# Splitting the gate, up and down pieces of early tiles between runs of small products in a delta-rule attention kernel with two expert layers

## Chip, cores and metric
The kernel runs on one core of one Trainium2 chip. The metric is the device time of one execution in microseconds. Engines: PE is TensorE, ACT ScalarE, DVE VectorE, POOL GpSimd, SP SyncE, which issues the DMAs. PEld is PE's weight load.

## What is computed
The reference has three stages, and the change touches the stretch in which the first and the second overlap.

```python
# attention: batch 4, heads 8, sequence 768, head width 48
y[t] = q[t] @ state
state = state + beta[t] * outer(k_n[t], v[t] - state^T k_n[t])
# first expert layer: x [3072, 384], 8 experts, inner width 1024
P = sinkhorn(exp(x @ w_gate - max))            # 8 rounds
out = sum_e P[:, e] * (relu(x @ w1[e]) @ w2[e])
# second layer: inner width 2048
h = out @ w_in;  result = (h * cos(h)) @ w_out
```

## The kernel before
**Attention.** The sequence is worked in 6 groups (g = 0 to 5) of 4 steps (c = 0 to 3, called step 0 to step 3 here); a step takes 64 positions of 8 heads and 2 batches. Groups 0 to 2 are one pair of batches, 3 to 5 the other, so the state starts anew in group 3. A step on PE (`step`, L645) is a list of runs of small products (32 or 64 products each), written out by hand: `L657` keys by state, then `L681` the correction (needs the residual R from DVE, L1530), `L482` query products of the next step, `L698` queries by state (needs W, which ACT copies at L976), `L704` the state update (ACT copies it at L1036 as S), `L709` the outputs (ACT copies them at L1045 as yT). In some steps merges of triangular blocks, `L492` and `L495`, 64 small products each, are called as well (`merge`, L499); their results are copied by ACT at L1003 (Y1) and L1007 (X). The last step of groups 2 and 5 has no L704, the first of groups 0 and 3 no L657 and no L698.

**Triangular inverses.** DVE works the inverse of the blocks of a later group column by column (`leaf`, L1465, lines L1479 and L1481), in every step but step 2, where it turns the result with two transposes (L1523, L1524) and then the next group's blocks (L1457). DVE's stream is in order: in step 3 it is R and the mask (L1538), `early_lo(g-1, 1)`, the norms and the leaf's start (L1423 to L1463), `early_lo(g-1, 2)`, and only then the columns of the leaf; R of the next step stands behind those.

**Early tiles.** From group 1, step 2 on, PE also works the first expert's first half for the tile of 512 tokens that the group before has finished, in pieces of large products (128x128 by 512): up pieces j = 0 to 3 (`early_up`, L551, 9 products), the gate (`early_gate`, L567, 9), and down pieces d = 0 to 2 (`early_down`, L585, 12). Where they stand is written out in three functions: `beside_residual` (L610, between L657 and L681), `beside_update` (L631, called at L684 after L482 and ahead of the merges) and `beside_outputs` (L638, after L709). After an up piece ACT makes hhi (L1062) from the bank, DVE makes hlo (L1547) from both, and only then is the one bank h_ps free for the next up piece. Up piece j of tile g-1: j = 0 in step 2, j = 1 and 2 in step 3, j = 3 in step 0 of the next group.

Of ACT's stream the lines L1165 to L1173 count: in steps 2 and 3 the copies hhi (j = 0, or j = 2) come ahead of the merge's copy X, of S and of yT.

**After it.** The early tiles end at 325 us, and from there to the end (the other expert passes and the second layer, L771 on) PE works through large products alone.

Of the kernel before, what the change touches and what calls it, by code (L numbers as in the profile page):

```python
# [77 lines left out]
def build(nc, kta, kqt, krow, vrow, brow, wcat, wgate, out):  # L78
# [371 lines left out]
    def _(pe):  # L450
# [100 lines left out]
        def early_up(t, j):  # L551
            if j == 0:
                pe.wait_ge(o["x_done"], t + 1)

                pe.wait_ge(s["wlo_done"], NT // 2)

            pe.wait_ge(o["h_done"], t * CH + j)
            if t == 0 and j == 0:

                pe.wait_ge(a["a_evac"], 4 * NG)  # L560
            for d in range(DC):
                pe.matmul(h_ps[:, :], w1(whi, 0, d, j), xt_hi[:, d, :], start=(d == 0), stop=False)
                pe.matmul(h_ps[:, :], w1(whi, 0, d, j), xt_lo[:, d, :], start=False, stop=False)
                mm = pe.matmul(h_ps[:, :], w1(wlo, 0, d, j), xt_hi[:, d, :], start=False, stop=(d == DC - 1))
            mm.then_inc(o["up_done"], 1)

        def early_gate(t):  # L567
# [4 lines left out]
            for d in range(DC):  # L572
# [3 lines left out]
            mm.then_inc(o["gate_done"], 1)  # L576
# [8 lines left out]
        def early_down(t, d):  # L585
            if d == 0:
                pe.wait_ge(o["h_done"], (t + 1) * CH)

                pe.wait_ge(s["wlo_done"], NT)
# [9 lines left out]
            for j in range(CH):  # L599
# [3 lines left out]
            mm.then_inc(o["down_done"], 1)  # L603
# [26 lines left out]

        def beside_update(g, c):  # L631

            if g >= 1 and c == 2:
                early_up(g - 1, 0)
            if g >= 1 and c == 3:
                early_up(g - 1, 2)

        def beside_outputs(g, c):  # L638

            if g >= 2 and c == 0:  # L640
                early_gate(g - 2)
            if g >= 2 and c == 1:
                early_down(g - 2, 1)

        def step(g, c):  # L645
# [38 lines left out]
            beside_update(g, c)  # L684
# [8 lines left out]
            if c == 3 and g + 1 < NG:  # L693
                merge(g + 1, 1)
            pe.wait_ge(a["w_evac"], i + 1)
# [4 lines left out]
            if not last:  # L700
# [5 lines left out]
                mm.then_inc(a["ku_done"], 1)  # L706
            pe.wait_ge(a["p_evac"], i + 1)
# [211 lines left out]
    def _(act):  # L919
# [215 lines left out]
        for g in range(NG):  # L1135
            near, far = g + 1 < NG, g + 2 < NG
            for c in range(STEPS):
# [25 lines left out]
                elif c == 0:  # L1163
                    merged(g, 3)
                if c == 2 and g >= 1:  # L1165
                    early_hi(g - 1, 0)
                if c == 3:
                    if g >= 1:
                        early_hi(g - 1, 2)
                    if near:  # L1170
                        merged(g + 1, 1)
                state(g, c)
# [725 lines left out]
```

## Time and profile before

| what | us |
|---|---|
| median of 3 runs | 2217.0 |
| lowest, highest | 2215.49, 2217.49 |
| the profiled execution | 2215.68 |
| its span | 2213.9 |
| PE busy in it | 2169.7 (98%) |
| DVE, ACT, POOL busy | 1019.6, 702.7, 507.2 |
| granted TensorE clock, mean | 0.985 |

The profiled execution took 1.3 us less than the median; 1.8 us of it lie around its span. Of the span the stretch from 118.5 us (the first early up piece) to 311.6 us (the last attention product) is the one that holds the instructions that the change moves. In a timeline row the columns are start, duration, engine, line, operation, output and inputs, shape, count, and in brackets the idle time before and what ended it; "issue" there means that the engine waited for nothing that the profile shows.

### The profile page before, as it was taken

The page shows a single profiled execution, that of the slowest core. Times are in us where ns is not written, and L with a number is a line of the kernel's source. Part 1 is how long each engine was busy: PE and PEld are TensorE (multiplying, and loading weights), DVE is VectorE, ACT ScalarE, POOL GpSimd, SP SyncE. Part 2 cuts the span into 40 slices and gives each one's busy share as a digit, 9 for nine tenths or more (in the row PEclk, how much of TensorE's full clock was granted, in tenths as well). Part 3 has the DMA queues.
Part 4 walks back from the last instruction along what each step waited for, and adds up shares of the span by engine and source line. Part 5 has one row for each costly group of instructions (what it writes and reads, how often), then busy time and mean ns, then how long its engine had stood idle before and what let it go on. Part 6 is the DMA issues. An engine that isn't in the chain of part 4 may idle for free.

```text
span 2213.9 us, 41130 instructions
## 1 busy us (share of the span) xinstructions
PE 2169.7 (98%) x15885; PEld 1793.8 (81%) x15885; DVE 1019.6 (46%) x1724; ACT 702.7 (32%) x1197; POOL 507.2 (23%) x409
## 2 busy tenths in 40 slices
PE   8798999999999999999999999999999999999999
PEld 7777778888888888888888888888888888888887
DVE  8898726432322323223223232232322347777777
ACT  4655543111111111111111111111111237666665
POOL 1000010045332322323323233232332330000000
PEclk6899999999999999999999999999999999999999
DMA  5434332021111111111111101111111100000001
GB/s 140 121 91 119 104 117 74 24 54 43 29 33 29 29 40 36 32 30 28 33 28 28 47 28 33 28 30 32 28 35 42 29 24 15 15 15 15 0 15 71
DMA packets 83116, 97.74 MB, mean 44 GB/s; under 512 B 6848, under 2 KB 68608, under 8 KB 83008
## 3 DMA queue, kind: packets, MB, share of 16 engines
q1 hardware_dynamic: 83008, 96.18, 16.0%
q8 instruction: 82, 1.34, 0.3%
q14 instruction: 26, 0.21, 0.0%
HBM read 82.69 MB, written 8.75 MB: 41 GB/s over the span
## 4 chain that ended last, share of the span: by engine, by line
PE 91%; DVE 6%; issue 1%; ACT 1%; DMA 0%; SPq 0%; DVEq 0%; ACTq 0%
PE h L774 7%; PE h L776 7%; PE h L775 7%; PE p_h L774 7%; PE p_h L776 7%; PE p_h L775 7%; PE am_y L812 4%; PE am_y L813 4%; PE am_y L814 4%; PE cy_y_y L812 4%; PE cy_y_y L813 4%; PE cy_y_y L814 4%; PE o_y L812 2%; PE o_y L813 2%; PE state_y L814 2%; PE state_y L812 2%
## 5 line engine op out<-in xcount | busy, mean ns | idle before, releaser
L1384 POOL TENSOR_TENSOR acc<-acc,py 128x512 f32 (+1 forms) x252 | 324.1, 1318 | 746.2 <-DVE py L1732 746.2
L1244 ACT ACTIVATE hhi<-h 128x512 fp32r<-128x512 f32 x182 | 109.0, 599 | 769.7 <-PE h L776 769.7
L1695 DVE SCALAR_TENSOR_TENSOR hlo<-h,hhi 128x512 fp32r<-128x512 f32 x182 | 125.9, 692 | 473.5 <-ACT hhi L1244 473.5
L1695 DVE SCALAR_TENSOR_TENSOR hlo<-p_h,hhi 128x512 fp32r<-128x512 f32 x182 | 125.8, 691 | 404.3 <-ACT hhi L1244 404.3
L1346 POOL TENSOR_TENSOR wlo<-stage,whi (+1 forms) x114 | 146.8, 1289 | 630.1 <-ACT whi L1089 605.2
L774 PE MATMUL p_h<-xhi,whi 128*128 (+1 forms) x690 | 269.1, 390 | 0.6 <-DVE scr L1792 0.6
L774 PE MATMUL h<-xhi,whi 128*128 (+1 forms) x690 | 268.9, 390 | 0.0
L776 PE MATMUL h<-xhi,wlo 128*128 (+1 forms) x690 | 268.7, 389 | 0.0
L776 PE MATMUL p_h<-xhi,wlo 128*128 (+1 forms) x690 | 268.7, 389 | 0.0
L775 PE MATMUL p_h<-xlo,whi 128*128 (+1 forms) x690 | 268.6, 389 | 0.0
L775 PE MATMUL h<-xlo,whi 128*128 (+1 forms) x690 | 268.6, 389 | 0.0
L1244 ACT ACTIVATE hhi<-p_h 128x512 fp32r<-128x512 f32 x182 | 109.0, 599 | 435.4 <-PE p_h L776 435.4
L774 PEld LDWEIGHTS p_h<-xhi,whi 128*128 128x128 f32 x690 | 129.6, 188 | 27.7 <-DVE scr L1792 1.0
L776 PEld LDWEIGHTS h<-xhi,wlo 128*128 128x128 f32 x690 | 129.7, 188 | 26.8
L776 PEld LDWEIGHTS p_h<-xhi,wlo 128*128 128x128 f32 x690 | 129.6, 188 | 26.9
L775 PEld LDWEIGHTS h<-xlo,whi 128*128 128x128 f32 x690 | 129.6, 188 | 26.8
L774 PEld LDWEIGHTS h<-xhi,whi 128*128 128x128 f32 x690 | 129.6, 188 | 26.7
L775 PEld LDWEIGHTS p_h<-xlo,whi 128*128 128x128 f32 x690 | 129.6, 188 | 26.7
L812 PE MATMUL am_y<-hhi,whi 128*128 128x512 f32 x368 | 143.3, 389 | 0.0
L813 PE MATMUL am_y<-hlo,whi 128*128 128x512 f32 x368 | 143.2, 389 | 0.0
L814 PE MATMUL am_y<-hhi,wlo 128*128 128x512 f32 x368 | 143.2, 389 | 0.0
L812 PE MATMUL cy_y_y<-hhi,whi 128*128 128x512 f32 x364 | 141.9, 390 | 0.0
(279 smaller groups left out, 3820.6 us busy)
## 6 DMA issues: line engine op xcount, KB each, us to landing
stage<-wcat SPq DMA_DIRECT2D x38, 768.0 KB, 4.4
pb<-p_scratch SPq DMA_DIRECT2D x84, 256.0 KB, 4.7
kq<-kqt SPq DMA_DIRECT2D x48, 192.0 KB, 3.5
v<-vrow SPq DMA_DIRECT2D x24, 192.0 KB, 3.7
kb<-krow SPq DMA_DIRECT2D x24, 192.0 KB, 3.8
acc<-yT SPq DMA_DIRECT2D x144, 32.0 KB, 2.3
kT<-kta SPq DMA_DIRECT2D x20, 192.0 KB, 4.3
acc<-y_scratch SPq DMA_DIRECT2D x5, 768.0 KB, 4.7
```

Of the source, the lines that this page charges most:

```text
L774: pe.matmul(hps[bank][:, 0:TILE], w1(whi, buf, d, j), x_h, start=(d == 0), stop=False)
L775: pe.matmul(hps[bank][:, 0:TILE], w1(whi, buf, d, j), x_l, start=False, stop=False)
L776: mm = pe.matmul(hps[bank][:, 0:TILE], w1(wlo, buf, d, j), x_h, start=False, stop=(d == DC - 1))
L812: pe.matmul(y, w2(whi, half, j, d), hhi[:, j, :], start=(j == 0), stop=False)
L813: pe.matmul(y, w2(whi, half, j, d), hlo[:, j, :], start=False, stop=False)
L814: mm = pe.matmul(y, w2(wlo, half, j, d), hhi[:, j, :], start=False, stop=(j == CH - 1))
L1244: act.activation(hhi[:, j, :], hps[j % 2][:, 0:TILE], ACT.Relu).then_inc(s["hhi_done"], 1)
L1346: pool.tensor_tensor(wlo[buf][:, c], stage[:, c], whi[buf][:, c].bitcast(F32), ALU.subtract).then_inc(s["wlo_done"], 1)
L1384: pool.tensor_tensor(y, y, py[:, d, :], ALU.add).then_inc(s["added"], 1)
L1695: dve.scalar_tensor_tensor(out=hlo[:, j, :], in0=hps[j % 2][:, 0:TILE], scalar=0.0, in1=hhi[:, j, :].bitcast(F32), op0=ALU.max, op1=ALU.su ...
```

## The change
The three helpers take a range of their products, `lo` to `hi`; only the last part counts up the semaphore, and some waits are met again by the second part. `beside_update` is called later, after the merges and just ahead of the wait for W. A new function `beside_state` stands between L704 and L709.

In step 0 (groups 2 to 5) the gate's first 3 products go in ahead of L698, the other 6 stay after L709. In step 1 the first 3 products of down piece 1 go between L704 and L709, the other 9 stay. In steps 2 and 3 (groups 1 to 5) the first 6 products of up piece 0, or 2, go ahead of L698 and the last 3 between L704 and L709. In step 3 the merge L495 comes ahead of them. On ACT, hhi of these two pieces is copied after X and S. DVE, POOL and SP are as before.

```diff
--- before.py
+++ after.py
@@ -548,8 +548,8 @@
             merge_units(0, 1, am_ps[0], c * HEADS, (c + 1) * HEADS).then_inc(a["m_done"], 1)
 
 
-        def early_up(t, j):
-            if j == 0:
+        def early_up(t, j, lo=0, hi=DC):
+            if j == 0 and lo == 0:
                 pe.wait_ge(o["x_done"], t + 1)
 
                 pe.wait_ge(s["wlo_done"], NT // 2)
@@ -558,22 +558,24 @@
             if t == 0 and j == 0:
 
                 pe.wait_ge(a["a_evac"], 4 * NG)
-            for d in range(DC):
+            for d in range(lo, hi):
                 pe.matmul(h_ps[:, :], w1(whi, 0, d, j), xt_hi[:, d, :], start=(d == 0), stop=False)
                 pe.matmul(h_ps[:, :], w1(whi, 0, d, j), xt_lo[:, d, :], start=False, stop=False)
                 mm = pe.matmul(h_ps[:, :], w1(wlo, 0, d, j), xt_hi[:, d, :], start=False, stop=(d == DC - 1))
-            mm.then_inc(o["up_done"], 1)
-
-        def early_gate(t):
+            if hi == DC:
+                mm.then_inc(o["up_done"], 1)
+
+        def early_gate(t, lo=0, hi=DC):
 
             pe.wait_ge(s["gate_lo"], 1)
 
             pe.wait_ge(o["evac"], OUTS * t if t < EARLY else OUTS * (t - 1) + 2)
-            for d in range(DC):
+            for d in range(lo, hi):
                 pe.matmul(o_ps[0:N_EXP, :], wgr[:, d, 0, :], xt_hi[:, d, :], start=(d == 0), stop=False)
                 pe.matmul(o_ps[0:N_EXP, :], wgr[:, d, 0, :], xt_lo[:, d, :], start=False, stop=False)
                 mm = pe.matmul(o_ps[0:N_EXP, :], wgr[:, d, 1, :], xt_hi[:, d, :], start=False, stop=(d == DC - 1))
-            mm.then_inc(o["gate_done"], 1)
+            if hi == DC:
+                mm.then_inc(o["gate_done"], 1)
 
         def early_logits(t):
 
@@ -582,8 +584,8 @@
                 mm = pe.transpose(o_ps[:, b * N_EXP:(b + 1) * N_EXP], lgT[0:N_EXP, b * P:(b + 1) * P], ident8[0:N_EXP, :])
             mm.then_inc(s["logits_done"], 1)
 
-        def early_down(t, d):
-            if d == 0:
+        def early_down(t, d, lo=0, hi=CH):
+            if d == 0 and lo == 0:
                 pe.wait_ge(o["h_done"], (t + 1) * CH)
 
                 pe.wait_ge(s["wlo_done"], NT)
@@ -596,11 +598,12 @@
             else:
                 pe.wait_ge(a["y_evac"], NS)
             bank = early_bank(t, d)
-            for j in range(CH):
+            for j in range(lo, hi):
                 pe.matmul(bank[:, :], w2(whi, 0, j, d), hhi[:, j, :], start=(j == 0), stop=False)
                 pe.matmul(bank[:, :], w2(whi, 0, j, d), hlo[:, j, :], start=False, stop=False)
                 mm = pe.matmul(bank[:, :], w2(wlo, 0, j, d), hhi[:, j, :], start=False, stop=(j == CH - 1))
-            mm.then_inc(o["down_done"], 1)
+            if hi == CH:
+                mm.then_inc(o["down_done"], 1)
 
         def unread(n, bank):
 
@@ -628,19 +631,31 @@
             if g >= 1 and c == 3:
                 early_up(g - 1, 1)
 
+
         def beside_update(g, c):
 
+            if g >= 2 and c == 0:
+                early_gate(g - 2, 0, 1)
             if g >= 1 and c == 2:
-                early_up(g - 1, 0)
+                early_up(g - 1, 0, 0, 2)
             if g >= 1 and c == 3:
-                early_up(g - 1, 2)
+                early_up(g - 1, 2, 0, 2)
+
+        def beside_state(g, c):
+
+            if g >= 2 and c == 1:
+                early_down(g - 2, 1, 0, 1)
+            if g >= 1 and c == 2:
+                early_up(g - 1, 0, 2)
+            if g >= 1 and c == 3:
+                early_up(g - 1, 2, 2)
 
         def beside_outputs(g, c):
 
             if g >= 2 and c == 0:
-                early_gate(g - 2)
+                early_gate(g - 2, 1)
             if g >= 2 and c == 1:
-                early_down(g - 2, 1)
+                early_down(g - 2, 1, 1)
 
         def step(g, c):
             first, last = is_first(g, c), is_last(g, c)
@@ -681,7 +696,6 @@
                 mm = pe.matmul(rows(chain_all, b)[:, par, n, :], rows(X, b ^ par)[:, g % 2, c * HEADS + h, :], r, start=True, stop=True)
             mm.then_inc(a["w_done"], 1)
             query_products(i + 1)
-            beside_update(g, c)
             if (g, c) == (0, 0):
                 first_merge(1)
                 joins(2)
@@ -692,6 +706,7 @@
                 merge(g, 3)
             if c == 3 and g + 1 < NG:
                 merge(g + 1, 1)
+            beside_update(g, c)
             pe.wait_ge(a["w_evac"], i + 1)
             if not first:
                 for h, par, n, b in fours:
@@ -704,6 +719,7 @@
                         mm = pe.matmul(rows(state_ps, b, HD)[:, h * HD:(h + 1) * HD], rows(kb, b)[:, c, h, :],
                                        rows(W, b)[:, h, :], start=(first and h == 0), stop=False, skip_group_check=True)
                 mm.then_inc(a["ku_done"], 1)
+            beside_state(g, c)
             pe.wait_ge(a["p_evac"], i + 1)
             for h, par, n, b in fours:
                 mm = pe.matmul(rows(y_all, b ^ par, HD)[:, par, n, :], rows(W, b)[:, h, :], rows(P_, b)[:, i % 2, h, :], start=False,
@@ -1162,14 +1178,14 @@
                     first_merged(3)
                 elif c == 0:
                     merged(g, 3)
+                if c == 3 and near:
+                    merged(g + 1, 1)
+                state(g, c)
+
                 if c == 2 and g >= 1:
                     early_hi(g - 1, 0)
-                if c == 3:
-                    if g >= 1:
-                        early_hi(g - 1, 2)
-                    if near:
-                        merged(g + 1, 1)
-                state(g, c)
+                if c == 3 and g >= 1:
+                    early_hi(g - 1, 2)
                 outputs(g, c)
 
                 if c == 0 and g >= 2:
```

## Rows read from the trace of the kernel before

**Rows 1.** The page, part 4: shares of the chain that ended last, by engine.
```profile
PE 91%; DVE 6%; issue 1%; ACT 1%; DMA 0%; SPq 0%; DVEq 0%; ACTq 0%
```

**Rows 2.** Busy time by engine (us, instructions), granted clock, DMA in two stretches.
```profile
118.50:242.97 124.47, 112.03 (x2951) 89.65 (x2951) 111.13 (x250) 66.53 (x115) 3.80 (x3) 1.00 0.38 102
242.97:311.60 68.63, 64.96 (x1641) 52.28 (x1640) 28.91 (x51) 31.45 (x53) 3.78 (x3) 0.98 0.38 106
```

**Rows 3.** PE waits, 119 to 311 us: who waited for whom: us, times, longest.
```profile
PE cy_y_y L681 <- DVE R L1530: 4.7, 4, 2.1
PE h L562 <- DVE hlo L1547: 2.7, 3, 1.1
PE state_y L704 <- issue: 1.7, 2, 1.0
...
PE cy_y_y L709 <- issue: 1.3, 3, 0.6
PE am_y L492 <- issue: 1.1, 2, 0.7
PE am_y L495 <- issue: 0.8, 1, 0.8
...
PE cy_y_y L657 <- issue: 0.6, 1, 0.6
```

**Rows 4.** Busy time between two neighbouring issue waits, columns as in 2.
```profile
227.49:236.08 8.59, 7.59 (x255) 6.46 (x256) 8.04 (x21) 4.61 (x8) 0.00 (x0) 1.00 0.46 108
```

**Rows 5.** Timeline of PE, group 3, step 2: start, us, count.
```profile
209.44 0.50 PE L562 MATMUL h<-xhi,whi 128*128 128x512 f32 x1
...
209.78 0.39 PE L563 MATMUL h<-xlo,whi 128*128 128x512 f32 x1
...
211.39 0.39 PE L564 MATMUL h<-xhi,wlo 128*128 128x512 f32 x1
...
211.71 0.66 PE L698 MATMUL cy_y_y<-kq,S 48*48 48x64 f32 x32
...
212.83 0.26 PE L709 MATMUL cy_y_y<-P__75,W 64*48 64x64 f32 x2
```

**Rows 6.** Timeline of ACT: the copy W of the same step.
```profile
211.12 0.49 ACT L976 ACTIVATE W<-cy_y_y 128x384 f32<-128x384 f32 x1
```

**Rows 7.** Timeline of DVE, group 3 (step 2), group 1 (step 2), idle before in brackets.
```profile
121.54 0.69 DVE L1547 SCALAR_TENSOR_TENSOR hlo<-h,hhi 128x512 fp32r<-128x512 f32 x1 [0.52 <-ACT hhi L1062]
...
205.00 0.56 DVE L1530 TENSOR_TENSOR R<-v,cy_y_y 128x384 f32<-128x384 f32 x1 [0.69 <-PE cy_y_y L657]
...
213.52 0.68 DVE L1547 SCALAR_TENSOR_TENSOR hlo<-h,hhi 128x512 fp32r<-128x512 f32 x1
```

**Rows 8.** Timeline of ACT, group 3, step 3.
```profile
218.41 0.60 ACT L1003 ACTIVATE stage<-am_y 128x512 f32<-128x512 f32 x1
218.91 0.59 ACT L1062 ACTIVATE hhi<-h 128x512 fp32r<-128x512 f32 x1
```

**Rows 9.** Timeline of DVE, the same step.
```profile
219.53 0.69 DVE L1547 SCALAR_TENSOR_TENSOR hlo<-h,hhi 128x512 fp32r<-128x512 f32 x1 [1.64 <-ACT hhi L1062]
...
223.59 0.69 DVE L1547 SCALAR_TENSOR_TENSOR hlo<-h,hhi 128x512 fp32r<-128x512 f32 x1
```

**Rows 10.** Timeline of PE, the same step: merge products after the up piece.
```profile
222.54 1.20 PE L495 MATMUL am_y<-stage 32*32 32x32 f32 x64
```

**Rows 11.** Timelines of DVE and PE, group 4, step 1.
```profile
241.98 0.55 DVE L1530 TENSOR_TENSOR R<-v,cy_y_y 128x384 f32<-128x384 f32 x1
...
242.97 0.68 PE L681 MATMUL cy_y_y<-R,X 64*64 64x48 f32 x32
```

**Rows 12.** Timeline of PE, and granted clock of two stretches, columns as in 2.
```profile
94.71 1.76 PE L482 MATMUL p_h<-kq 48*64 48x64 f32 x27 [2.07 <-issue]
...
95.00:100.00 5.00, 5.00 (x145) 4.82 (x143) 4.58 (x13) 1.17 (x2) 0.00 (x0) 0.50 0.25 51
260.00:265.00 5.00, 4.77 (x55) 3.40 (x58) 1.16 (x2) 2.21 (x5) 0.00 (x0) 0.66 0.98 286
```

## The prediction

> **What bounds the kernel now.** I read the chain that ended last first: PE carries 91% of it, DVE 6% [rows 1]. Nothing behind the early tiles is touched, and there PE works without a break, so whatever the end of the attention stretch gains or loses is the change's worth in the total. The reader should then see that the stretch has two halves. Up to 242.97 us DVE is busy 111.1 of 124.5 us (89%), after it 28.9 of 68.6 us (42%) [rows 2]. PE's waits say the same: 4.7 us for R and 2.7 us for hlo, both DVE's, beside 5.5 us of "issue" (1.7 + 1.3 + 1.1 + 0.8 + 0.6), where no semaphore is missing [rows 3]. The issue waits have a pattern. Between two neighbouring ones, at 227.49 and 236.08 us, stand 255 matmuls and 256 weight loads, 511 instructions [rows 4], and the others lie at multiples of such a distance, each inside a long stretch of small products. I read them as waits for the next block of the instruction stream: small products use it up faster than it comes. That is what the change bears on, as large products between them give it time.
>
> **What an issue wait is worth.** In the first half DVE hands over late, so a wait of PE that goes there is mostly found again as a longer wait for R; I count 0. The one exception is step 2 of group 3: DVE there idles 0.69 us for the keys by state [rows 7], behind an issue wait of 0.6 us (in the L709 entry [rows 3]), so that one is worth 0.6. In the second half lie two, one in the L492 entry (0.7) and the one in L495 (0.8) [rows 3]: 1.5 us on the path.
>
> **The splits themselves.** An up piece starts at 209.44, its second product 0.34 later; the last starts at 211.39 and the small products follow 0.32 later. Between them the pace is (211.39 - 209.78) / 7 = 0.23 [rows 5]. So a piece costs 0.11 + 0.09 = 0.20 us beyond its products, and each split pays that once more: 6 products take 1.58 us, 3 take 0.89 instead of 2.27 together. The repeated waits are met when they come and cost nothing.
>
> **Step 2: hlo(0) comes later.** Today up piece 0 ends at 211.71 and W is copied from 211.12 to 211.61 [rows 5, 6]. After it, 6 products end at 209.44 + 1.58 = 211.02 and PE stands until W is there at 211.67. Then the L698 and L704 runs, 212.83 - 211.71 = 1.12 us [rows 5], to 212.79, and the last 3 products to 213.68. Hhi (0.60, [rows 8]) ends at 214.4, so hlo(0) starts there and not at 213.52 [rows 7]: 0.9 us later. In group 1 DVE already stands waiting for hhi (0.52 us, [rows 7]), so there the whole 1.12 + 0.20 = 1.3 us count. For group 2 I take 1.2, between the two. Hlo(0) matters since values, the block transpose, the next R and the chain over ACT to hhi(1) all stand behind it in DVE's queue, and hlo(1) waits for that chain (1.64 us idle, [rows 9]), so the delay passes on in full.
>
> **Step 3: hlo(2) comes later still.** Take M = 218.41 + 0.60 = 219.01, the end of Y1; hhi(1) follows, hlo(1) ends at 219.53 + 0.69 = 220.22, and DVE reaches hlo(2) at 223.59 without a gap [rows 8, 9]. Now the merge L495, 1.20 us [rows 10], starts at M + 0.05 and fills the wait for hlo(1): good, but it only fills. 6 products run 220.27 to 221.85, L698 and L704 to 222.97, 3 products to 223.86, hhi to 224.6. Hlo(2) starts 1.0 us later than today. Behind it on DVE stand the values, all columns of the leaf and R of the next step; DVE has no gap there. In group 2 L704 is missing, 0.65 us of the 1.12, which leaves 0.35.
>
> **The sum.** Group 1: 1.3 + 1.0 = 2.3, which L681 of group 2 in steps 0 and 1 inherits, since it waits for R today. Group 2: + 1.2 + 0.35 = 3.85. Group 3: the exception above gives back 0.6 less 0.2 for the down split, then + 0.9 + 1.0 = 5.35. In group 4, step 1, R is made from 241.98 to 242.53 and L681 starts at 242.97 [rows 11]: 0.45 of slack, leaving 4.9. From there the splits: down and up in two groups, 5 x 0.20 + 0.1 for the gate (it pays only the 0.09) = 1.1. In the last step hlo(2) has lost the L698 run, 0.48 us, as cover before up piece 3 and PE waits that longer: 0.5. Less the two issue waits, 1.5. Together 4.9 + 1.1 + 0.5 - 1.5 = 5.0 us. The clock enters twice. It fell at 260 to 265 us (0.66 of full, so 5 x 0.34 = 1.7 us lost, [rows 12]) behind a long stretch of small products, which the change breaks up: worth 0 to 1.7. Against it the waits for R grow: by the same reckoning (today's share of the 4.7 us [rows 3], plus DVE's delay, less PE's own slip) PE stands some 3.5 us at group 2, step 0, 4 us at group 3, step 1, and 3.4 us at group 4, step 0. Behind an idle of 2.07 us the trace has 95 to 100 us at 0.50, the lower level of 1.2 GHz [rows 12]. One such fall costs 0 where DVE still bounds, up to 1.7 where it doesn't. I take half of each, so they cancel.
>
> The sum stands against the profiled execution, 2215.7 us (span 2213.9 and 1.8 around it): 2220.7. That execution is 1.3 us under the median; on the median it is 2217.0 + 5.0 = **2222.0 us**. ACT's new order costs nothing: X and S are copied before hhi's products are even done. SP's y_done, y_evac and its moves shift with the steps, with no new wait; POOL has nothing here.
>
> **A rule weighed.** The row shows 511 instructions from one issue wait to the next [rows 4] and 0.6 to 1.0 us lost at each [rows 3]. The Trainium skill ("Runtime: NRT & Kernel Launch", Instruction fetch mechanics) says the stream comes in blocks of 256 instructions and that crossing to a new one is mostly hidden. The distance agrees, the "hidden" does not. By the page these waits would be something else and would stay, and the sum would be 5.0 + 1.5 + 0.6 = 7.1 us. I go by the row.
>
> **Rivals.** *PE's own waits decide, faster.* If DVE's delays don't reach R (because hlo(0) and hlo(2) have slack that I don't see), all 5.5 us of issue go and the merge covers 1.8 of the 2.7 us for hlo (two thirds: one of the three waits is in group 5, which has no such merge), less 18 splits (14 x 0.20 + 4 x 0.09 = 3.2): -4.1, and with the clock's 1.7 -5.8, so 2211 to 2213 us. It decides at the point where up piece 2 ends before 222.9, 0.7 us ahead of DVE's arrival at 223.59 [rows 9]; I find 223.86. For it: issue is the largest kind. Against it: DVE runs without a gap between hlo(1) and R. *Near no change.* The delays come at half their size (hhi earlier, the block transpose waiting for something else anyway): 2.7 - 0.4 in place of 4.9, so 2.3 + 1.1 + 0.5 - 1.5 = 2.4, with the clock's 1.7 gained about +0.7: 2217.7 to 2219.4. *The clock falls in the new idle stretches*, and the 1.7 is not won back: 5.0 + 0.85 + up to 3 x 1.7 where not hidden, say two: 2225 to 2226. The Trainium skill ("TensorE: Matmul & The Clock Gate", HAM oscillation) says waits inside a kernel make PE's clock drop so that the work after each starts slow. Rows 12 agree at one place. *The blocks fall badly*: new issue waits in runs of 256 instructions that stay whole; each under 0.5 us and half of them hidden, so + 0.5 to 1; inside the range.
>
> **Chances.** Forecast (DVE's queue delayed, 2220 to 2224): 0.5. Near no change: 0.25. Faster by PE's waits: 0.1. Clock: 0.15. The measurement tells 0.2%, 4.4 us, from no change, so "slower" begins at 2221.4, just under my forecast: of the 0.5 some 0.38 lie above it, and the clock case's 0.15 with it: slower 0.53. Same 0.37. Faster (under 2212.6) 0.10. The range leaves out the faster case and the worst of the clock: 2214.5 to 2226.0.
>
> **What would show it.** Right: the issue waits between 119 and 311 us fall from 5.5 to under 2; waits of L681 for R rise from 4.7 to over 10 us, with single ones of 3 us and more; DVE gets new idle time before hlo(2) in step 3 (about 1 us in groups 1 and 3) behind hhi; the wait for hlo before up piece 2 is gone in groups 1 to 4; L698 waits about 0.6 us for W in groups 2 and 3; the last attention product ends 4 to 6 us later. Wrong: R is not later against the start of its group, or the L681 waits stay near 5 us; then the removed issue waits are a gain. If the L681 waits grow and the end doesn't move, a cover in the second half was misjudged.

## Result, and the profile after

The changed kernel takes 2227.15 us (median of 6 runs, 2224.89 to 2230.81), the kernel before 2217.21 (6 runs beside them, 2215.49 to 2220.20). The ratio is 1.0048, 95% interval 1.0037 to 1.0059: slower by 0.5%, as forecast in sign, but 5 us above the forecast of 2222.0 and 1.2 us outside its range. The profiled execution took 2227.21 us, span 2225.5. Of all the runs told of below one, of the kernel with both orders, took 3092 us at a mean granted clock of 0.65, for no reason that is known; its ratio leaves it out.

The page of the changed kernel, parts 1 and 4: busy time by engine, and the chain that ended last.
```profile
PE 2177.6 (98%) x15885; PEld 1796.3 (81%) x15885; DVE 1019.8 (46%) x1724; ACT 703.0 (32%) x1197; POOL 507.2 (23%) x409
...
PE 92%; DVE 4%; ACT 2%; issue 1%; SPq 1%; DMA 0%; DVEq 0%; ACTq 0%
```
Against [rows 1] DVE's share is 4% instead of 6% and ACT's 2% instead of 1%; the chain now runs through ACT's copy of hhi(2) in groups 1 to 3, as it did not before. (Lines moved: R is L1546, the keys by state L672, the products that wait for R L696, those that wait for W L713, the state L719, hhi L1078, hlo L1563.)

PE's waits, 119 to 311 us, to be read beside [rows 3]: who waited for whom, us, times, longest.
```profile
PE cy_y_y L696 <- DVE R L1546: 11.5, 3, 4.6
...
PE cy_y_y L713 <- ACT W L992: 1.5, 2, 0.9
PE state_y L719 <- issue: 0.4, 1, 0.4
PE am_y L495 <- issue: 0.3, 1, 0.3
```
The issue waits have gone from 5.5 to 0.7 us and the waits for hlo before up piece 2 are gone in groups 2 and 3, as the change would have it (that of group 5, 0.8 us, now falls at 318.96 us, behind this window). The wait for R has gone from 4.7 to 11.5 us, in three waits instead of four. What made R late stands in the timeline of DVE, here group 1 step 3 and group 3 (idle time before an instruction in brackets).
```profile
134.17 0.69 DVE L1563 SCALAR_TENSOR_TENSOR hlo<-h,hhi 128x512 fp32r<-128x512 f32 x1 [1.32 <-ACT hhi L1078]
...
221.14 0.69 DVE L1563 SCALAR_TENSOR_TENSOR hlo<-h,hhi 128x512 fp32r<-128x512 f32 x1 [0.95 <-ACT hhi L1078]
...
227.17 0.69 DVE L1563 SCALAR_TENSOR_TENSOR hlo<-h,hhi 128x512 fp32r<-128x512 f32 x1 [1.64 <-ACT hhi L1078]
...
233.16 0.69 DVE L1563 SCALAR_TENSOR_TENSOR hlo<-h,hhi 128x512 fp32r<-128x512 f32 x1 [1.97 <-ACT hhi L1078]
```
In [rows 7, 9] hlo(0) of group 3 (213.52) and hlo(2) (223.59) have no bracket at all. Now DVE stands for hhi before both; the wait for hhi(1) is the old one (1.64). These are the idle times that the forecast announced, with about 1 us each for hlo(2) of groups 1 and 3; 1.32 and 1.97 us came.

The granted clock is the second thing that changed. Three windows of the changed kernel (start:end, length, then busy time with instructions of PE, PEld, DVE, ACT, POOL, the granted clock, the DMA share, GB/s), and PE's timeline at its three waits for R:
```profile
142.02:148.85 6.83, 6.82 (x159) 5.40 (x153) 6.52 (x16) 1.66 (x3) 0.00 (x0) 0.50 0.14 28
...
200.00:206.80 6.80, 4.70 (x128) 4.71 (x128) 6.35 (x17) 0.49 (x1) 0.00 (x0) 0.51 0.01 4
241.00:247.80 6.80, 6.79 (x159) 5.37 (x153) 6.35 (x17) 1.66 (x3) 0.00 (x0) 0.50 0.16 31
```
```profile
141.50 0.69 PE L696 MATMUL cy_y_y<-R,X 64*64 64x48 f32 x32 [3.47 <-DVE R L1546]
142.20 1.97 PE L482 MATMUL p_h<-kq 48*64 48x64 f32 x32
...
202.10 0.68 PE L696 MATMUL cy_y_y<-R,X 64*64 64x48 f32 x16 [4.57 <-DVE R L1546]
...
240.49 0.69 PE L696 MATMUL cy_y_y<-R,X 64*64 64x48 f32 x32 [3.47 <-DVE R L1546]
```
PE idles 3.47, 4.57 and 3.47 us for R (forecast: 3.5, 4 and 3.4), and the clock falls from 2.4 to 1.2 GHz for 6.8 us each time, within the second of these waits (from about 200.1 us) and 0.5 us behind the end of the other two; in the kernel before it had been full from 118.5 to 242.97 us [rows 2].

**Where the time went.** R is made once a step, so the distance from one R to the next says what each step costs and leaves out where the stretch began (that wanders before anything that the change touches: R of step 1.2 starts at 109.92 us in the changed kernel, at 112.78 before, and between 109.9 and 113.6 over all kernels here). Worked out from the starts of R in the timelines of DVE; "1.3" is group 1, step 3; the forecast's terms are beside them.
```
from:to    before  after  after-before  forecast
1.3:2.0     13.61  14.86     +1.25       +1.0   hlo(2), group 1
2.0:2.1     13.47  13.46      0           0
2.1:2.2      8.13   8.60     +0.47        0     clock
2.2:2.3     11.69  13.20     +1.51       +1.2   hlo(0), group 2
2.3:3.1     24.76  25.34     +0.58       +0.35  hlo(2), group 2
3.1:3.2      8.64  10.06     +1.42       -0.4   clock
3.2:3.3     11.74  12.83     +1.09       +0.9   hlo(0), group 3
3.3:4.0     13.58  15.50     +1.92       +1.0   hlo(2), group 3
4.0:4.1     11.66  11.65      0           0
4.1:4.2      7.99  10.40     +2.41       -0.25  clock; slack 0.45, down split 0.2
4.2:5.3     54.57  53.40     -1.17       -0.6   splits, issue waits, old dip
sum        179.84 189.30     +9.46
```
Behind it the last hlo is 0.35 us later still, so from R of 1.3 on it is 9.8 us, where the forecast had 5.0 - 1.3 = 3.7.

The first term, 1.3 us for hlo(0) of group 1, this pair of executions can't show. Counted from the start of the span hlo(0) starts 1.24 us later (122.78 against 121.54), but that the two figures are alike is chance: from the first product of up piece 0 to hlo(0) it is 5.96 us instead of 2.97, and the piece had started 1.75 us earlier. Part of the 3.0 us is a fall of the clock from 118.2 to 121.5 us, behind a wait of 1.73 us of PE for ACT. At full clock throughout, this distance is 2.96 to 2.98 us with a whole piece (three kernels) and 4.48 with a split one (the kernel with both orders, below): 1.5 us for the split, the 1.3 of the forecast and the 0.15 more that a split turns out to cost.

The spans of the two profiled executions differ by 11.6 us and the medians by 9.9, since the profiled execution of before was 1.5 us under its median.

### The profile page after: what moved, and what is told of

It is laid out like the page before. It is cut to its first block, busy times and chain, and to the rows that moved or that the text cites. A ratio compares the mean times of both kernels' runs of the same rounds, so it can differ in the third digit from the quotient of the medians.

```text
span 2225.5 us, 41135 instructions
## 1 busy us (share of the span) xinstructions
PE 2177.6 (98%) x15885; PEld 1796.3 (81%) x15885; DVE 1019.8 (46%) x1724; ACT 703.0 (32%) x1197; POOL 507.2 (23%) x409
## 4 chain that ended last, share of the span: by engine, by line
PE 92%; DVE 4%; ACT 2%; issue 1%; SPq 1%; DMA 0%; DVEq 0%; ACTq 0%
PE h L790 7%; PE h L792 7%; PE h L791 7%; PE p_h L790 7%; PE p_h L792 7%; PE p_h L791 7%; PE am_y L828 4%; PE am_y L829 4%; PE am_y L830 4%; PE cy_y_y L828 4%; PE cy_y_y L829 4%; PE cy_y_y L830 4%; PE o_y L828 2%; PE state_y L828 2%; PE o_y L829 2%; PE state_y L829 2%
```

## The experiments

In each, the ratio is to the kernel before, timed beside it; its median was 2215.7 us beside the last kernel, 2216.9 beside four (smaller doses, all splits with the old order of ACT, and the two that have both orders) and 2216.5 beside the other eight. Steps are named as in the table above. Code that is left out is marked by "...".

### What makes hhi late: the place of the products, the order of ACT, or both

**Only ACT's new order, in the kernel before.**
```
+                if c == 3 and near:
+                    merged(g + 1, 1)
+                state(g, c)
+
                 if c == 2 and g >= 1:
                     early_hi(g - 1, 0)
-                if c == 3:
-                    if g >= 1:
-                        early_hi(g - 1, 2)
-                    if near:
-                        merged(g + 1, 1)
-                state(g, c)
+                if c == 3 and g >= 1:
+                    early_hi(g - 1, 2)
                 outputs(g, c)
```


> The kernel before with ACT's new order alone: hhi of up pieces 0 and 2 behind the merge's copy X and behind S; PE is untouched, nothing is split. Theory A (what makes hlo late is where hhi stands in ACT's in-order queue, behind S, which waits for the whole L704 run): in step 3 hhi(2) waits for the merge, L698 and L704, so hlo(2) comes 2.0 to 2.7 us later in groups 1 to 3 and hlo(0) 0.8 to 1.8 us later, and with no split anywhere the time is as bad as the change or nearly: 2224 to 2229 us. Theory D as I wrote it (the last three products of the split pieces are what comes late, ACT's order costs nothing): 2216 to 2218 us.


Measured: 2233.36 us (2230.75 to 2235.62), ratio 1.0070 (1.0057 to 1.0083): some 16 us slower, more than the whole change and 4 us above the range expected. The timeline of DVE, groups 1 and 2:
```profile
125.16 0.69 DVE L1547 SCALAR_TENSOR_TENSOR hlo<-h,hhi 128x512 fp32r<-128x512 f32 x1 [3.25 <-ACT hhi L1062]
...
139.35 0.69 DVE L1547 SCALAR_TENSOR_TENSOR hlo<-h,hhi 128x512 fp32r<-128x512 f32 x1 [4.09 <-ACT hhi L1062]
...
191.27 0.69 DVE L1547 SCALAR_TENSOR_TENSOR hlo<-h,hhi 128x512 fp32r<-128x512 f32 x1 [2.14 <-ACT hhi L1062]
```
In group 1 the last product of up piece 2 starts at 135.40 us; X is copied from 136.97, S from 138.27 and only then, from 138.66, hhi(2). Its copy stands in ACT's queue behind two that come later, and DVE waits 2.1 to 4.1 us before hlo(2), where it had waited for nothing. Not all of the 16 us is this: the clock is at 1.2 GHz for 31 us of this stretch, in five falls, against 20 us in the three long falls of the changed kernel. What those cost here was not taken apart.

**The up pieces whole again, gate and down split, ACT's new order kept.** (The calls ahead of L698 make all nine products, the calls behind the state go; the merge still stands ahead of up piece 2.)
```
             if g >= 1 and c == 2:
-                early_up(g - 1, 0, 0, 2)
+                early_up(g - 1, 0)
             if g >= 1 and c == 3:
-                early_up(g - 1, 2, 0, 2)
+                early_up(g - 1, 2)
...
-            if g >= 1 and c == 2:
-                early_up(g - 1, 0, 2)
-            if g >= 1 and c == 3:
-                early_up(g - 1, 2, 2)
```


> The changed kernel with up pieces 0 and 2 whole again ahead of L698 (up piece 2 still after the merge L495); the gate and the down piece stay split. Theory D: hlo(0) and hlo(2) come nearly as early as before (hlo(2) by the cover of the merge), so the waits for R are back near 5 us and no clock falls follow: 2216 to 2219 us. Theory S: 10 of 18 splits gone, so a bit over half of the 10 us: 2221 to 2222 us.


Measured: 2227.78 us (2225.77 to 2228.96), ratio 1.0051 (1.0038 to 1.0065). The theory expected to hold missed by 9 us and its rival by 6. Both had overlooked the order of ACT, which the next run puts back.

**The same, with hhi copied ahead of S again** (behind X).
```
                 if c == 3 and near:
                     merged(g + 1, 1)
-                state(g, c)
-
                 if c == 2 and g >= 1:
                     early_hi(g - 1, 0)
                 if c == 3 and g >= 1:
                     early_hi(g - 1, 2)
+                state(g, c)
                 outputs(g, c)
```


> The changed kernel with up pieces 0 and 2 whole (gate and down piece split, L495 ahead of up piece 2), and on ACT hhi ahead of S again, behind X. It differs from the run with whole ups only in that order on ACT. Theory A: hlo(2) comes when DVE reaches it, the waits for R are back near 5 us, 2216 to 2219 us. If the gate and down splits and the merge's new place are to blame for what the run with whole ups still lost, it stays at 2225 or more.


Measured: 2218.98 us (2214.91 to 2221.82), ratio 1.0011 (1.0002 to 1.0020): seven and a half of the ten us are back.

**All splits, with hhi copied ahead of S again** (the same edit on ACT, in the changed kernel).


> The changed kernel with all its splits, but with ACT's copy of hhi(0) and hhi(2) ahead of the copy of the state S again. Theory (hhi is late since its last products are late on PE, and S is copied while they run, so that ACT's order is hidden in the changed kernel): hhi starts no earlier, hlo(2) still idles over 1 us in groups 1 and 3, and S now stands behind hhi, some 1 us later, so PE waits for S: 2227 to 2232 us. Rival (ACT's order alone, which costs 17 us without the splits, is what makes the changed kernel slow): 2217 to 2222 us.


Measured: 2229.23 us (2227.26 to 2231.38), ratio 1.0060 (1.0048 to 1.0072). In the timeline of ACT the copy of hhi(2) in group 1 waits for PE's last products, and S behind it waits for nobody:
```profile
133.77 0.60 ACT L1078 ACTIVATE hhi<-h 128x512 fp32r<-128x512 f32 x1 [2.61 <-PE h L564]
134.26 0.48 ACT L1052 ACTIVATE S<-state_y 128x384 f32<-128x384 f32 x1
```
With the changed kernel itself these make a square of four: hhi is late for either of two reasons, since its last three products run behind the state (the split), or since its copy stands behind S (the order). Each alone holds it up (2229.2 and 2227.8 us, both together 2227.2), and only without either is most of the loss gone (2219.0). The forecast's "ACT's new order costs nothing" holds beside the splits and only beside them.

**Gate and down whole, up pieces split.**
```
-            if g >= 2 and c == 0:
-                early_gate(g - 2, 0, 1)
...
-            if g >= 2 and c == 1:
-                early_down(g - 2, 1, 0, 1)
...
             if g >= 2 and c == 0:
-                early_gate(g - 2, 1)
+                early_gate(g - 2)
             if g >= 2 and c == 1:
-                early_down(g - 2, 1, 1)
+                early_down(g - 2, 1)
```


> The changed kernel with the gate and down piece 1 whole again after L709; both up pieces stay split. Theory D: the delay of DVE's queue comes from the up pieces alone, so nearly all of it stays: 2225 to 2228 us (less 4 x 0.2 to 0.4 for the down pieces, plus issue waits that come back in steps 0 and 1). Theory S: 8 of 18 splits gone: 2222 to 2223 us.


Measured: 2226.96 us (2224.84 to 2227.71), ratio 1.0046 (1.0032 to 1.0059), as the whole change. PE's waits, 119 to 311 us:
```profile
PE cy_y_y L692 <- DVE R L1542: 9.8, 3, 3.5
PE state_y L715 <- issue: 1.5, 2, 1.0
...
PE cy_y_y L721 <- issue: 0.8, 1, 0.8
```
The up pieces, with the order of ACT that goes with them, carry the loss.

Some 2.5 us of issue wait are back, all before R of 4.1, and from R of 1.3 to R of 4.1 it takes 125.55 us against 125.50. But it would be wrong to call these waits worth nothing. One of 0.99 us in step 3.0 is (2.3:3.1 takes 25.36 us, 25.34 without it). One of 0.80 us in step 2.1 makes 2.1:2.2 9.22 us instead of 8.60, and one of 0.54 in step 3.3 makes 3.3:4.0 15.67 instead of 15.50; what offsets them is a fall of the clock at 205 us that lasts 3.4 us instead of 6.8 (3.1:3.2 is 9.27 us, not 10.06).

Which issue waits count, the other kernels show. In step 2.0 none does: 2.0:2.1 is 13.45 to 13.47 us in all fifteen kernels, with an issue wait of 1.17 us in it or with none. In step 2.1 nearly all of it does: where the clock stays full and the wait is none, 0.17, 0.72, 1.05 and 1.28 us, 2.1:2.2 is 8.11, 8.13, 8.68, 9.06 and 9.27 us. The wait of 1.28 us (in the kernel with the change only from group 4 on, below) and the R behind it:
```profile
158.87 0.33 PE L730 MATMUL cy_y_y<-P__75,W 64*48 64x64 f32 x9 [1.28 <-issue]
162.90 0.55 DVE L1552 TENSOR_TENSOR R<-v,cy_y_y 128x384 f32<-128x384 f32 x1 [1.32 <-PE cy_y_y L675]
```
In this step DVE's work is done about when PE's keys come (it idles 0.15 us even where PE never stands), so a wait of PE goes straight into R; step 3.1 is the same (8.57 to 8.64 us with 0.55 to 0.60 us of issue wait, 8.10 without).

### Is it DVE's queue that passes the delay on?

**The changed kernel, with DVE's work put where it would otherwise stand.** In groups 1 to 3 hlo(0) goes behind the values and the block transpose, hlo(2) behind the first four columns of the leaf.
```
-                    if g >= 1:
+                    if g >= 1 and not far:
                         early_lo(g - 1, 0)
...
-                    if g >= 1:
+                    if g >= 1 and not far:
                         early_lo(g - 1, 2)
...
                 if c == 2 and far:
                     leaf_start(g + 2)
+                    if g >= 1:
+                        early_lo(g - 1, 0)
...
                 if far and c == 3:
-                    leaf(*COLS[c])
+                    leaf(COLS[c][0], 5)
+                    if g >= 1:
+                        early_lo(g - 1, 2)
+                    leaf(5, COLS[c][1])
```


> The changed kernel with one edit on DVE: in step 2 hlo(0) stands behind the values and the block transpose, in step 3 hlo(2) stands behind the values and the first four columns of the leaf (groups 1 to 3). PE's order is that of the change. Theory D (the delay comes through DVE's in-order queue: DVE stands for hhi before hlo(0) and hlo(2), and R, which stands behind them, comes late; the clock falls behind the long waits for R): the idle time of DVE before hlo goes in groups 1 to 3, the waits of PE for R fall from 11.5 to under 7 us, and the time falls from 2227 to 2218 to 2222 us. Theory S (the 18 splits cost PE its time by themselves): the order on DVE changes nothing, 2226 to 2228 us.


Measured: 2219.05 us (2215.04 to 2222.57), ratio 1.0012 (1.0003 to 1.0021). Some seven and a half of the ten lost us are back, with every split and ACT's order in place. PE's waits of that run, 119 to 311 us:
```profile
PE cy_y_y L696 <- DVE R L1546: 5.4, 4, 2.0
PE h L562 <- DVE hlo L1563: 2.1, 3, 0.8
```
The longest wait for R is 2.0 us instead of 4.6, and steps 2.2:2.3 and 3.2:3.3 are 11.70 and 11.60 us, where the kernel before has 11.69 and 11.74. So the loss came through hlo standing in DVE's queue ahead of the work for R.

**The change only from group 4, step 1, on,** where DVE has time.
```
+        def late(g, c):
+            return (g, c) >= (4, 1)
...
```
(`late` decides in each place that the change touches, on PE and on ACT.)


> The change made only from group 4, step 1 on, where DVE has time to spare; the steps before are as in the kernel before, on PE and ACT. If DVE's lateness in groups 1 to 3 makes the loss, this one is within 2 us of the kernel before (six splits at 0.2 to 0.4 us and 0.5 us in the last step, less up to 1.5 us of issue waits and part of a fall of the clock): 2216.5 to 2218.5 us. If the splits cost PE by themselves, a third of the loss shows: 2220 us.


Measured: 2217.18 us (2213.98 to 2218.70), ratio 0.9999 (0.9991 to 1.0008): no difference. The loss comes from what the change does before that point.

### What the clock's falls cost

**Unread products in the three long waits for R.** The changed kernel with large products that stand ahead of L696 and write a merge bank that is free, so that PE is not idle.
```
+            if (g, c) in FILL:
+                pe.wait_ge(a["m_evac"], 4 * g + 2)
+                unread(FILL[g, c], am_ps[0])
...
+FILL = {(2, 0): 13, (3, 1): 18, (4, 0): 13}
```


> The changed kernel with products nobody reads (128x512, into a merge bank that is free) ahead of the three long waits for R: 13, 18 and 13 of them at 0.23 us, so 3.0, 4.1 and 3.0 us of work in waits of 3.47, 4.57 and 3.47 us. Nothing else moves. If the falls of the clock (6.8 us each behind those waits) are what lies between the forecast of 2222 and the measured 2227, they go, and the time is 2221 to 2224 us. If DVE's lateness alone makes the time, it stays at 2226 to 2228 us.


Measured: 2227.15 us (2226.25 to 2231.50), ratio 1.0056 (1.0042 to 1.0069): missed in the total. The three falls are gone, and steps 3.1:3.2 and 4.1:4.2 take 8.11 and 8.42 us instead of 10.06 and 10.40. But a new one begins at 154.3 us and makes step 2.1:2.2 11.02 us instead of 8.60, and there are 2.8 us of issue waits, one of them (1.15 us) ahead of hhi(2) in group 3, where 3.3:4.0 takes 16.25 us instead of 15.50. The window of the new fall (columns as above), and PE's timeline there:
```profile
154.30:161.10 6.80, 6.79 (x143) 5.72 (x135) 6.18 (x21) 0.98 (x2) 0.00 (x0) 0.50 0.02 5
```
```profile
153.78 0.69 PE L700 MATMUL cy_y_y<-R,X 64*64 64x48 f32 x32 [1.89 <-DVE R L1550]
154.47 1.86 PE L483 MATMUL p_h<-kq 48*64 48x64 f32 x30
...
157.06 1.52 PE L723 MATMUL state_y<-W,kb 64*48 64x48 f32 x32
```
**The same with smaller doses and a fourth place,** `FILL = {(2, 0): 10, (2, 1): 6, (3, 1): 14, (4, 0): 10}`.


> The changed kernel with unread products in front of four waits for R, in smaller doses than in e6_fill: 10 at group 2 step 0, 6 at group 2 step 1, 14 at group 3 step 1 and 10 at group 4 step 0. Theory (each fall of the clock that PE's waits for R bring costs some 2 us of the changed kernel's time): with the four longest waits shortened, the clock stays at full from 120 to 300 us and the time is 2222 to 2224.5 us. Rival (the products use up the waits and the instruction stream falls behind elsewhere, or the clock's price is hidden by DVE): 2226 to 2229 us, with the clock at full or not.


Measured: 2224.78 us (2223.61 to 2226.36), ratio 1.0040 (1.0027 to 1.0053), 0.3 us above the range expected. The clock is full from 124 us to the end of the stretch. The windows in which it had fallen, and two neighbouring R of DVE:
```profile
142.00:148.85 6.85, 5.62 (x229) 4.64 (x229) 6.61 (x15) 2.17 (x5) 0.00 (x0) 1.00 0.23 47
200.00:206.80 6.80, 5.39 (x140) 4.51 (x138) 6.35 (x17) 0.49 (x1) 0.00 (x0) 1.00 0.05 19
241.00:247.80 6.80, 6.49 (x218) 4.43 (x213) 6.28 (x17) 2.85 (x5) 0.00 (x0) 1.00 0.24 57
```
```profile
250.63 0.56 DVE L1550 TENSOR_TENSOR R<-v,cy_y_y 128x384 f32<-128x384 f32 x1
258.74 0.55 DVE L1550 TENSOR_TENSOR R<-v,cy_y_y 128x384 f32<-128x384 f32 x1 [0.15 <-PE cy_y_y L676]
```
And the same two in the changed kernel:
```profile
251.53 0.55 DVE L1546 TENSOR_TENSOR R<-v,cy_y_y 128x384 f32<-128x384 f32 x1
261.93 0.55 DVE L1546 TENSOR_TENSOR R<-v,cy_y_y 128x384 f32<-128x384 f32 x1 [2.46 <-PE cy_y_y L672]
```
8.11 us against 10.40: at half clock DVE waits 2.46 us for PE's keys before it can make R, at full clock 0.15. From R of 1.3 to R of 5.3 the run needs 184.71 us, the changed kernel 189.30: 4.6 us, of which 0.5, 2.0 and 2.3 lie in the three steps behind the three waits. As total times the two kernels aren't told apart with certainty (their intervals against the kernel before overlap, and this execution came to R of 1.3 1.7 us later than the changed kernel's); the distances tell them apart. They repeat: without a fall step 4.1:4.2 took 7.99 to 8.70 us in ten kernels, with one 10.00 to 10.56 in five.

### Does the change win with its delays mended, and which version is best

**ACT's copy of hhi(1) ahead of the second half of the scatter and of Y1, in the kernel before.** DVE waits 1.64 us for it in group 3 [rows 9] and 1.65 in groups 1 and 2.
```
-                if c == 3 and g >= 1:
+                if c == 3 and g == NG - 1:
                     early_hi(g - 1, 1)
...
                     if c == 2 and far:
                         root(g + 2)
+                    if c == 2 and g >= 1:
+                        early_hi(g - 1, 1)
                     scatter(g + 1, c - 2, 2, 4)
                     merged(g + 1, 2 * (c - 2))
```


> The kernel before with one edit on ACT: hhi(1) stands ahead of the second half of the scatter in step 2 and of Y1. If the queue from hlo(1) through the leaf to R decides groups 1 to 3, hlo(1) comes 0.5 to 0.95 us earlier in each, and the time falls by 1 to 3 us, to 2213.5 to 2215.5. If PE decides, nothing moves.


Measured: 2214.14 us (2210.53 to 2216.90), ratio 0.9991 (0.9982 to 0.9999). The timeline of DVE in group 3: the wait is 0.32 us, not 1.64.
```profile
220.84 0.69 DVE L1549 SCALAR_TENSOR_TENSOR hlo<-h,hhi 128x512 fp32r<-128x512 f32 x1 [0.32 <-ACT hhi L1062]
```
It is the quickest of all, though 2.4 us is at the edge of what can be told, and its profiled execution has a fall of the clock of 6.8 us at 197.6 us.

**That and DVE's order of the earlier experiment, in the kernel before.**


> The kernel before with two new orders: ACT copies hhi(1) ahead of the second half of the scatter and of Y1 (as in e11_hhi1_first), and DVE makes hlo(0) behind values and block transpose and hlo(2) behind four columns of the leaf (as in e5_dve_order). Theory (DVE bounds groups 1 to 3, and each idle time of DVE in front of hlo is on the path): what e11_hhi1_first left of DVE's waits for hhi in groups 1 to 3 goes too, 0.5 to 1.5 us: 2212.5 to 2214.5 us. Rival (with hhi(1) early, PE bounds by its own instructions and issue waits): 2214 to 2217 us.


Measured: 2220.22 us (2214.99 to 2224.56), ratio 1.0012 (1.0002 to 1.0022): above both ranges, and worse by some 5 us than the one edit alone (0.9991). PE's waits, 160 to 200 us, and its timeline at up piece 1 of group 2:
```profile
PE h L562 <- DVE hlo L1549: 2.7, 2, 1.5
...
172.82 0.61 PE L562 MATMUL h<-xhi,whi 128*128 128x512 f32 x1 [1.16 <-DVE hlo L1549]
```
The up pieces share one bank, so up piece 1 waits until hlo(0) has been made; with hlo(0) put off, the piece, hhi(1) and hlo(1) are late (DVE then waits 3.57 us for it), and steps 2.3:3.1 and 3.3:4.0 take 26.68 and 15.05 us instead of 23.81 and 12.25.

**Both orders in the changed kernel.**


> The changed kernel (all splits, ACT's new order) with both orders of e15_hhi1_dve_order. If the delays that the splits bring to DVE are taken away by these orders, what is left is the splits' own price on PE less the issue waits that they remove. Theory (18 splits at 0.2 to 0.4 us against 5.5 us of issue waits, most of which DVE's bound hides): 2215 to 2219 us, some 2 to 4 us above e15_hhi1_dve_order. Rival (freed of DVE, the splits win the issue waits): under 2213 us and below e15_hhi1_dve_order.


Measured: 2223.71 us (without the one run named above 2218.51 to 2224.60), ratio 1.0030 (1.0020 to 1.0041), above both ranges. PE's waits, 119 to 243 us:
```profile
PE cy_y_y L696 <- DVE R L1548: 5.4, 4, 1.8
PE am_y L495 <- ACT stage L1019: 3.5, 3, 1.2
```
The change has put the merge ahead of up piece 2, and the merge reads Y1, which ACT now copies behind hhi(1). So as they stand, the splits with their merge and the early hhi(1) get in each other's way.

**The quickest version with the splits where DVE is free** (steps 1 and 2 of group 4, all of group 5).


> The kernel before with ACT's copy of hhi(1) ahead of the second half of the scatter and of Y1 (e11_hhi1_first, 2.4 us), and with the change's splits only in steps 1 and 2 of group 4 and in all of group 5. Step 3 of group 4 stays whole, since there the merge would wait for a Y1 that now stands behind hhi(1), as in e16_splits_both_orders. Theory (splits pay where DVE no longer bounds: issue waits and a fall of the clock go, 0 to 1 us): 2212.5 to 2215 us. Rival (a split costs 0.4 us or more of PE's time there, more than issue waits and clock give back): 2215 to 2217 us.


Measured: 2216.55 us (2214.18 to 2218.98), ratio 1.0006 (0.9997 to 1.0015): the rival. From R of step 4.1 to R of step 5.3 it takes 62.53 us, the version without splits 60.48. Of the 2.05 us, 0.69 lie in steps 5.1 and 5.2, one split each; 1.22 lie in steps 4.3 and 5.0, where it has 1.3 us of issue waits, so the splits did not even remove those, and the version without has 0.4. Splits don't pay where PE bounds either. The late change alone takes 61.86 us here and the kernel before 62.56, but the kernel before has the old dip of the clock at 261.5 us in it, worth some 1.3, and the version without splits avoids that too.

## Why the prediction was right in sign and short in size

**Right, with its terms.** DVE's queue decides, and each late hhi passes on in full: DVE idles for hhi 1.32, 1.37, 0.61, 0.95 and 1.97 us before hlo(2) of group 1, hlo(0) and hlo(2) of group 2 and of group 3, and the steps grow by 1.25, 1.51, 0.58, 1.09 and 1.92. PE's three waits for R were placed and sized within 0.6 us. W is waited for in two groups (0.92 and 0.56 us, forecast 0.6). The rival that PE's own waits decide is refuted by the waits for R (11.5 us, where it had them near 5) and by the order of DVE alone giving back seven and a half us, and the one of half delays by the table.

**Right in the sum, wrong as a rule: an issue wait in the first half counts 0, with step 3.1 as the one exception.** Step 3.1 gave back 0.5 us as forecast (8.64 against 8.10), but step 2.1 is of the same kind and step 3.3 ahead of hhi(2) is too in the changed kernel, as the experiments show. It cost the sum little, since the kernel before had only 0.17 us of issue wait in step 2.1. The pattern was also read too neatly: from 200.99 to 227.49 us there are 1271 matmuls and weight loads, which is no multiple of 511 but close to one of half that, and the single waits run from 0.17 us to 0.99, not from 0.6. Why PE stands there is inferred from this spacing; no run here tries it.

**Failed: "I take half of each, so they cancel"** (the clock). Three falls of 6.8 us came, one within and two right behind a long wait for R, and cost 0.49 + 1.96 + 2.29 = 4.7 us, by the distance to the run with the smaller doses, which has none of them; the dip that went had cost some 1.3 (step 4.3:5.0 is 12.23 us with it and 10.91 in the quickest version without). Net +3.4 us where 0 stood. The rival with the clock (2225 to 2226 us, chance 0.15) was the nearest to what happened, and still 1 us short. The reckoning behind it, half the length at half clock, 1.7 us for a fall, was taken from a fall of 3.4 us; these lasted 6.8. The first costs little: DVE takes the same 13.46 us from R of 2.0 to R of 2.1 with it and without. The other two lie in steps where DVE has little to do and waits for PE's keys.

**Failed: "each split pays that once more", 0.20 us.** It costs 0.35. Steps 5.1:5.2 and 5.2:5.3 hold one split each, the down piece and up piece 0. The starts of R in group 5 before (first fence) and after (second):
```profile
283.90 0.56 DVE L1530 TENSOR_TENSOR R<-v,cy_y_y 128x384 f32<-128x384 f32 x1 [6.42 <-PE cy_y_y L657]
294.48 0.55 DVE L1530 TENSOR_TENSOR R<-v,cy_y_y 128x384 f32<-128x384 f32 x1 [8.96 <-PE cy_y_y L657]
304.54 0.56 DVE L1530 TENSOR_TENSOR R<-v,cy_y_y 128x384 f32<-128x384 f32 x1 [1.40 <-PE cy_y_y L657]
```
```profile
293.99 0.55 DVE L1546 TENSOR_TENSOR R<-v,cy_y_y 128x384 f32<-128x384 f32 x1 [5.55 <-PE cy_y_y L672]
304.92 0.55 DVE L1546 TENSOR_TENSOR R<-v,cy_y_y 128x384 f32<-128x384 f32 x1 [9.31 <-PE cy_y_y L672]
315.33 0.55 DVE L1546 TENSOR_TENSOR R<-v,cy_y_y 128x384 f32<-128x384 f32 x1 [0.24 <-PE cy_y_y L672]
```
10.58 and 10.06 us became 10.93 and 10.41: +0.35 twice. Over the fifteen kernels step 5.1:5.2 has the one value or the other within 0.03, by whether its down piece is split; step 5.2:5.3 does too (10.06 or 10.41) in twelve, and the other three, 10.46 to 10.67, are those whose ACT order doesn't fit PE's place of the products. Where the missing 0.15 lies, the timeline of PE shows (changed kernel, group 3, step 2):
```profile
218.21 0.66 PE L713 MATMUL cy_y_y<-kq,S 48*48 48x64 f32 x32 [0.56 <-ACT W L992]
218.70 0.89 PE L719 MATMUL state_y<-W,kb 64*48 64x48 f32 x32
219.51 0.50 PE L562 MATMUL h<-xhi,whi 128*128 128x512 f32 x1
219.85 0.40 PE L563 MATMUL h<-xlo,whi 128*128 128x512 f32 x1
220.09 0.39 PE L564 MATMUL h<-xhi,wlo 128*128 128x512 f32 x1
220.41 0.66 PE L725 MATMUL cy_y_y<-P__75,W 64*48 64x64 f32 x32
```
The 0.11 at the first product (0.34 for 0.23) and the 0.09 behind the last (0.32 for 0.23) are there as forecast. But from the state's start to the first large product it is 0.81 us; from the state's start to the next small run it had been 0.64 to 0.67 (212.19 to 212.83 us before). The way out of the state's run into the large products costs 0.16 as well, and the forecast had looked only at the product's own start. (Out of the merge L495 it costs nothing: from its start to the next run it is 1.13 us, be that L698 or the up piece.) With 0.15 more in the five late hhi behind R of 1.3 and in the seven splits of the second half, that is some 1.8 us.

**The rest.** The slack of 0.45 us at step 4.1 was not seen again: without a fall the step takes 8.11 us, not less than before. Hlo(2) of group 3 idles 1.97 us, where 1.0 was forecast. In its timeline stands one new issue wait of 0.42 us in the state, ahead of the last three products. Without such a wait the idle time is 1.31 and 1.42 us (smaller doses; all splits with the old order of ACT), with waits of 0.42, 0.54 and 1.15 us it is 1.97, 2.13 and 2.68: each passes on its length and some 0.25 more. What the 0.25 is stays open.

From R of 1.3 on the forecast had 3.7 us and the trace shows 9.8. Of the 6.1 between them 3.4 are the clock, some 1.8 the splits, 0.45 the slack and 0.66 the issue wait ahead of hhi(2); they add up to 6.3. In the medians the forecast of 5.0 met 9.9.

## What to carry to other kernels

Before a large product is split or moved, find who copies its result, and what is queued behind that copy's reader: here 1 us on PE became 1 us of an in-order DVE twice a group, and PE then waited long enough to lose its clock. Time an engine's order together with the place of the work it copies, since either alone can hold a result back and mending one shows nothing. And where a forecast finds new idle stretches of 3 to 5 us on PE, count a fall of the clock in each at what the work right behind it costs, rather than setting it off against a gain elsewhere. An issue wait of PE isn't worth nothing just because another engine bounds the stretch: look which handover lies behind it.

## What the runs showed of the hardware that was not expected

- Every wait of PE of 3.3 us or more between 130 and 311 us was followed by a fall of the clock, in all fifteen kernels (fourteen waits of 3.30 to 4.58 us; the falls last 3.4 to 10.2 us). By the length of a shorter wait nothing can be told: behind 1.63 us a fall came in one kernel (3.4 us long) and behind 2.21 us in two (6.8 us), while 2.13 and 2.91 us brought none in two others, and the kernel with the larger doses has its fall of 6.8 us behind a wait of 1.89 us. The price depends on the work behind: the queries' 32 products take 1.97 us at 1.2 GHz and 1.15 at full clock, a state run 1.52 instead of 0.89.
- Setting large products in behind the state's run costs PE 0.27 us (0.16 at the way in, 0.11 at the first product) and 0.09 at the way out, which is the 0.35 by which steps with one split grow; behind the merge's run the way in costs nothing.
- The unread products meant to keep the clock up came with 2.8 us of issue waits in one run and 1.1 in the next, with doses of 44 and 40, where the changed kernel has 0.7. What decides where such a wait falls was not tried.
